# Folding the state into the first-layer weights for two batches at once, with the raw weights streamed through a ring

## What is computed

```python
scores = x @ state.T / 8;   a  = softmax(scores);   xread = a @ state
scores2 = state @ x.T / 8;  a2 = softmax(scores2);  sread = a2 @ x
t = concat([xread, sread], axis=2)       # 544 rows a batch, 4352 in all, width 512
y = ((t @ w_a) * (t @ w_b)) @ w_out      # w_a, w_b: 512 x 1536, w_out: 1536 x 512
e = argmax(y @ w_gate)                   # one of 8 experts for each row
out = softmax(y @ w_gate)[e] * (relu(y @ w1[e]) @ w2[e])
```

## Time and profile before

| what | us |
|---|---|
| median of 3 runs | 1473.31 |
| lowest and highest run | 1472.83, 1474.9 |
| span of the profiled execution, first to last instruction | 1464.0 |
| first stage in the trace, to the start of the state batch | 836.7 |
| share of the span that PE is busy | 95% |
| share of the span for DVE, ACT, POOL | 43%, 38%, 20% |

### The profile page before, as it was taken

One profiled execution on the slowest core, in us unless ns is written; L12 is line 12 of the kernel. 1 busy time (PEld: TensorE's weight loads), 2 busy tenths in 40 slices (PEclk: granted clock), 3 DMA queues, 4 the chain that ended last, 5 costly groups with the idle time before them and its releaser, 6 DMA issues.

```text
span 1464.0 us, 22574 instructions
## 1 busy us (share of the span) xinstructions
PE 1398.0 (95%) x6994; PEld 1160.4 (79%) x6995; DVE 630.3 (43%) x978; ACT 551.8 (38%) x920; POOL 287.3 (20%) x277
## 2 busy tenths in 40 slices
PE   6999999999999999999999996799999999999996
PEld 4688888888888888888888795688787888888885
DVE  4566566566565565666665547211111111111110
ACT  2344545445444544544454532122222222222221
POOL 0000222221221322222222321111111111111120
PEclk9999999999999999999999997699999999999998
DMA  7101543444344334435344556851677774171110
GB/s 240 44 22 65 175 142 133 158 136 153 135 149 162 128 131 170 138 126 180 125 158 144 189 187 205 260 167 43 206 251 257 248 255 157 60 255 43 43 38 0
DMA packets 127087, 215.17 MB, mean 147 GB/s; under 512 B 47760, under 2 KB 47760, under 8 KB 127056
## 3 DMA queue, kind: packets, MB, share of 16 engines
q1 hardware_dynamic: 115888, 186.70, 38.4%
q0 software_dynamic: 6560, 19.67, 4.0%
q10 hardware_dynamic: 4608, 8.39, 1.6%
HBM read 129.78 MB, written 86.77 MB: 148 GB/s over the span
## 4 chain that ended last, share of the span: by engine, by line
PE 72%; DMA 16%; DVE 5%; ACT 2%; issue 2%; SPq 1%; POOL 1%; DVEq 0%; ACTq 0%; POOLq 0%
PE YB L1172 15%; PE OB L1298 12%; PE HB L1285 12%; DMA WS<-expert_halves 11%; PE BB L1158 7%; PE AB L1158 7%; PE FB L1133 7%; DMA expert_halves<-raw 3%; DMA raw<-in_moe_w 2%; PE FB L1113 2%; PE FB L1094 2%; PE HT L1307 2%; PE FB L1142 2%; POOL raw L509 1%; PE FB L1138 1%
## 5 line engine op out<-in xcount | busy, mean ns | idle before, releaser
L509 POOL TENSOR_TENSOR raw<-raw,hi 128x512 f32<-128x512 f32 x128 | 190.6, 1499 | 702.1 <-ACT hi L688 702.1
L1285 PE MATMUL HB<-WS,xgh 128*128 x656 | 210.5, 402 | 6.7 <-DMA WS<-expert_halves 6.7
L1298 PE MATMUL OB<-WS,hth 128*128 x656 | 206.6, 396 | 4.0 <-DVE htl L1058 2.8
L1058 DVE TENSOR_TENSOR htl<-HT,hth 128x1024 fp32r<-128x1024 f32 x41 | 50.2, 1225 | 299.4 <-ACT hth L715 299.4
L1172 PE MATMUL YB<-WOh,gh 128*128 128x512 f32 x408 | 163.1, 400 | 1.3 <-ACT y_sb L634 0.6
L1172 PE MATMUL YB<-WOh,gl 128*128 128x512 f32 x408 | 159.9, 392 | 0.0
L1172 PE MATMUL YB<-WOl,gh 128*128 128x512 f32 x408 | 159.2, 390 | 0.0
L1158 PE MATMUL BB<-ATh,SWB 128*128 128x512 f32 (+1 forms) x432 | 152.2, 388 | 0.0
L1158 PE MATMUL AB<-ATh,SWA 128*128 128x512 f32 (+1 forms) x432 | 150.0, 383 | 2.0 <-ACT gp L657 2.0
L1285 PEld LDWEIGHTS HB<-WS,xgh 128*128 128x128 f32 x656 | 122.9, 192 | 32.5 <-issue 7.7
L1298 PEld LDWEIGHTS OB<-WS,hth 128*128 128x128 f32 x656 | 120.3, 188 | 28.8 <-issue 5.1
(11 more groups left out here) (187 smaller groups left out, 2389.1 us busy)
## 6 DMA issues: line engine op xcount, KB each, us to landing
WS<-expert_halves SPq DMA_DIRECT2D x128, 512.0 KB
raw<-in_moe_w SPq DMA_DIRECT2D x128, 256.0 KB, 2.7
expert_halves<-hi SPq DMA_DIRECT2D x128, 256.0 KB, 2.5
expert_halves<-raw SPq DMA_DIRECT2D x128, 256.0 KB, 2.9
y_rows<-y_sb ACTq DMA_DIRECT2D x32, 256.0 KB, 2.9
xq<-in_x SPq DMA_DIRECT2D x60, 128.0 KB, 2.9
WA<-in_moe_w_a SPq DMA_DIRECT2D x3, 1024.0 KB, 9.9
WB<-in_moe_w_b SPq DMA_DIRECT2D x3, 1024.0 KB, 12.0
```

The source lines that it names most:

```text
L509: eng.tensor_tensor(raw[:, q % 2, :], raw[:, q % 2, :], hi[:, q % 2, :].bitcast(F32), ALU.subtract).then_inc(s["e_lo"], 1)
L1058: eng.tensor_tensor(htl[:, :, :], HT[:, :, :].rearrange("p a (k c) -> p (a k) c", c=P), hth[:, :, :].bitcast(F32), ALU.subtract).then_inc( ...
L1285: last = eng.matmul(HB[:, i, :], act[:, k, :], w, start=(k == 0 and m == 0), stop=(k == KC - 1 and m == 2))
L1298: last = eng.matmul(OB[:, :], act[:, k, :], w, start=(k == 0 and m == 0), stop=(k == FEC - 1 and m == 2))
```

## The change

It does five things. (1) The state of two batches (a *pair*) is laid into one block: chunk k now gives 2 batches x 2 heads x 32 = 128 useful rows. A fold is one chunk, 3 matmuls, and its result is copied to both batches' part of `SW` in two ops of 64 partitions on ACT and two on DVE; a pair takes 24 folds. (2) `WA`, `WB` are gone; each fold's 128x512 chunk of raw weights is loaded when needed into the two-slot ring `wr` (12 slots `wfirst` in the preamble). SP issues each of these loads in order among its others, after waiting until the chunk that held the slot has been split. (3) Pair 0 is folded in float32: 8 folds in the preamble, 16 in batch 0. (4) The preamble no longer runs a2t and sr of batch 0; they move into its steps 0 and 1. (5) xt copies move from DVE to ACT, the softmax of scores is cut in three (shift, exp, normalise) and spread, the product with BB is taken one place earlier on DVE. The raw weights for the state batch also come through the ring. The loop over batches is written out.

```diff
-    state_v = state.rearrange("b (g i) n d -> b i n g d", i=4)
-    wa_v = w_a.rearrange("(k p) (j c) -> j p k c", p=P, c=512)
-    wb_v = w_b.rearrange("(k p) (j c) -> j p k c", p=P, c=512)
+    state_v = state.rearrange("(q r) (g c i) n d -> r c i n q g d", r=2, c=2, i=2)
+    w_v = [w.rearrange("(k p) (j c) -> j k p c", p=P, c=512) for w in (w_a, w_b)]
...
-        lows = ExitStack()
-        WL = [sb(n, [P, KC, FF], F32R, lows) for n in ("WAL", "WBL")]
-        lows.close()
-        W = [sb(n, [P, KC, FF], F32, first) for n in ("WA", "WB")]
-        SW = [sb(n, [P, FC, 2 * G, P], F32R, first) for n in ("SWA", "SWB")]
...
+        SW = sb("SW", [P, FJ, 2, 2, 4, 2 * G, P], F32R, first)
...
-        wfh, wfl = (sb(n, [P, 2, 512], F32R, heads) for n in ("wfh", "wfl"))
+        wfh, wfl = (sb(n, [P, 512], F32R, heads) for n in ("wfh", "wfl"))
+        wr = sb("wr", [P, 2, 512], F32, heads)
...
-        REST = {(0, 3): ("fold", 8), (1, 3): ("fold", 9), (2, 3): ("fold", 10), (3, 3): ("fold", 11)}
-        HEADS = {(4, 0): ("st", 0), (4, 1): ("xt", 0), (4, 2): ("xt", 1), (4, 3): ("fold", 0), (5, 0): ("st", 1),
-                 (5, 2): ("s1", 0), (5, 3): ("fold", 1), (6, 2): ("s2", 0), (6, 3): ("fold", 2),
-                 (7, 1): ("a2t", 0), (7, 2): ("sr", 0), (7, 3): ("fold", 3), (8, 2): ("xt", 2), (8, 4): ("xt", 3),
-                 (8, 3): ("fold", 4), (9, 1): ("s1", 1), (9, 2): ("s2", 1), (9, 3): ("fold", 5),
-                 (10, 1): ("a2t", 1), (10, 2): ("sr", 1), (10, 3): ("fold", 6),
-                 (11, 1): ("a1t", 0), (11, 2): ("a1t", 1), (11, 3): ("fold", 7)}
+        HEADS = {(4, 0): ("xt", 0), (4, 2): ("xt", 1), (5, 0): ("s1", 0), (5, 2): ("s2", 0), (6, 2): ("a2t", 0),
+                 (7, 0): ("sr", 0), (8, 0): ("xt", 2), (8, 2): ("xt", 3), (9, 0): ("s1", 1), (9, 2): ("s2", 1),
+                 (10, 2): ("a2t", 1), (11, 0): ("sr", 1), (11, 1): ("a1t", 0), (11, 2): ("a1t", 1)}
+        BEGIN = {(0, 0): ("a2t", 0), (0, 2): ("sr", 0), (1, 0): ("a2t", 1), (1, 2): ("sr", 1)}
+        NORM = {(6, 4): 0, (10, 4): 1}
+        FOLD_BEGIN = ((0, 1), (0, 3), (1, 1), (1, 3), (2, 1), (2, 3), (3, 0), (3, 1),
+                      (3, 3), (4, 1), (4, 3), (5, 1), (5, 3), (6, 1), (6, 3), (7, 1))
+        FOLD_ODD = ((4, 1), (4, 3), (5, 3), (6, 1), (6, 3), (7, 1), (7, 3), (8, 3), (9, 1), (9, 3), (10, 1), (10, 3))
+        FOLD_EVEN = ((0, 3), (1, 1), (1, 3), (2, 1), (2, 3), (3, 1), (3, 3), (4, 3), (5, 1), (5, 3), (6, 3), (7, 1))
...
+        PER_PAIR = FJ * 2 * KC
+        FOLDS = PAIRS * PER_PAIR
+        PRE = (("st", 0, 0), ("xt", 0, 0), ("xt", 1, 0), ("xt", 2, 0), ("xt", 3, 0), ("s1", 0, 0), ("s1", 1, 0),
+               ("s2", 0, 0), ("s2", 1, 0), ("a1t", 0, 0), ("a1t", 1, 0))
+
+        RING = 16
...
+        def folds_of(b):
+
+            if b == 0:
+                return {k: KC * 2 + i for i, k in enumerate(FOLD_BEGIN)}
+            if b % 2:
+                return {k: PER_PAIR * (b // 2 + 1) + i for i, k in enumerate(FOLD_ODD)}
+            return {k: PER_PAIR * (b // 2) + 12 + i for i, k in enumerate(FOLD_EVEN)}
...
+        def splits_of(b):
+            return {k: v - FOLDS for k, v in folds_of(b).items()} if b >= B - 1 else {}
...
+        def ring_free(i):
+
+            a = RING + i
+            if a < PER_PAIR:
+                return s["fill_done"], next(n for n, e in enumerate(ORDER) if e[:2] == ("fold", a)) + 1
+            if a < FOLDS:
+                return s["wf_lo"], a - PER_PAIR + 1
+            return s["ws_lo"], a - FOLDS + 1
...
+            def load_ring(slot):
+
+                for i in range(2, RINGS):
+                    if used_at(i - 2) == slot:
+                        eng.wait_ge(*ring_free(i - 2))
+                        load_raw(RING + i)
...
-            bodies(eng, emit)
...
-                        for q in pieces_of(b, f):
-                            load_piece(b, q)
-                            if q and not (isinstance(b, int) and b == 0 and q == LEAD):
-                                store_piece(b, q - 1)
-                if expert_in(b):
-                    store_piece(b, pieces_of(b, FC - 1)[-1])
-
-            bodies(eng, emit)
+                    for place in range(2):
+                        if (f, place) in slots:
+                            load_ring(slots[f, place] - RING)
+                    for q in pieces_of(b, f):
+                        load_piece(b, q)
+                        if q and not (b == 0 and q == LEAD):
+                            store_piece(b, q - 1)
+                    for place in range(2, PLACES):
+                        if (f, place) in slots:
+                            load_ring(slots[f, place] - RING)
+                store_piece(b, pieces_of(b, FC - 1)[-1])
             store_y(eng, B, 0)
...
+            def high_folded(a, bank):
+                p, j, m, k = fold_of(a)
+                for side in range(2):
+                    r = rows_of(side, k)
+                    eng.activation(SW[r, j, side, m, :, 2 * (k // 2), :], bank[r, :].rearrange("p (f c) -> p f c", c=P),
                                    ACT.Copy).then_inc(s["sw_hi"], 1)
-                    if not (isinstance(b, int) and b < 0 and a < 7) and not last_fold(a, b):
-                        high_fold(*next_fold(a, b)[:2], b)
-
-            def high_fold(j, w, b):
-                if isinstance(b, int) and b < 0:
-                    eng.wait_ge(w_in[j], 32)
-                eng.activation(wfh[:, :, :], w, ACT.Copy).then_inc(s["wf_hi"], 1)
+
+            def high_fold(a):
+
+                src, done, value = raw_piece(a)
+                eng.wait_ge(done, value)
+                eng.activation(wfh[:, :], src, ACT.Copy).then_inc(s["wf_hi"], 1)
+
+            def fold(a, n):
+                eng.wait_ge(s["fill_done"], n + 1)
+                high_folded(a, FB[:, n % 2, :])
+                if PER_PAIR <= a + 1 < FOLDS:
+                    high_fold(a + 1)
...
+            def split(i):
+                _, j, m, k = fold_of(i)
+                src, done, value = raw_piece(FOLDS + i)
+                eng.wait_ge(done, value)
+                eng.wait_ge(s["b_done"], (B - 2 + m) * FC + 4 * j + 4)
+                eng.activation(state_part(j, m, k, 0), src, ACT.Copy).then_inc(s["ws_hi"], 1)
 
...
+            def low_folded(a, bank):
+                p, j, m, k = fold_of(a)
+                for side in range(2):
+                    r, c = rows_of(side, k), 2 * (k // 2)
+                    place = SW[r, j, side, m, :, :, :]
+                    eng.wait_ge(s["sw_hi"], 2 * a + side + 1)
+                    eng.tensor_tensor(place[:, :, c + 1, :], bank[r, :].rearrange("p (f c) -> p f c", c=P),
+                                      place[:, :, c, :].bitcast(F32), ALU.subtract).then_inc(s["sw_lo"], 1)
+
+            def low_fold(a):
+                src, _, _ = raw_piece(a)
+                eng.wait_ge(s["wf_hi"], a - PER_PAIR + 1)
+                eng.tensor_tensor(wfl[:, :], src, wfh[:, :].bitcast(F32), ALU.subtract).then_inc(s["wf_lo"], 1)
+
+            def fold(a, n):
+                low_folded(a, FB[:, n % 2, :])
+                if PER_PAIR <= a + 1 < FOLDS:
+                    low_fold(a + 1)
+
+            def split(i):
+                _, j, m, k = fold_of(i)
+                src, _, _ = raw_piece(FOLDS + i)
+                eng.wait_ge(s["ws_hi"], i + 1)
+                eng.tensor_tensor(state_part(j, m, k, 1), src, state_part(j, m, k, 0).bitcast(F32), ALU.subtract)\
...
+            def fold(a, bank):
+
+                p, j, m, k = fold_of(a)
+                if p == 0:
+                    src, done, value = raw_piece(a)
+                    eng.wait_ge(done, value)
+                    return eng.matmul(bank, st[:, k, :], src, start=True, stop=True)
+                eng.wait_ge(s["stl_ready"], p + 1)
+                eng.wait_ge(s["wf_lo"], a - PER_PAIR + 1)
+                for i, (part, w) in enumerate(((sth, wfh), (sth, wfl), (stl, wfh))):
+                    last = eng.matmul(bank, part[:, k, :], w[:, :], start=(i == 0), stop=(i == 2))
+                return last
```

751 lines of the change are left out of this document (387 added, 364 removed).

## The result

| | us | against before |
|---|---|---|
| before, median | 1473.62 (1472.83 to 1474.9) | |
| changed, median | 1498.62 (1492.48 to 1503.66) | ratio 1.017, 95% interval 1.0142 to 1.0199 |
| changed, profiled execution | 1492.48, span 1490.7 | |

A forecast was written before the change was run, and what follows sets the result against it. PE was taken to bound batches 1 to 6. Against the 1464.0 us span, -7.8 (preamble, batch 0), -51.6 (matmuls), +17.4 (stalls), -4.3 (batch 7) and +1.5 (state batch) gave 1419; 9.3 carried over made 1428.5, range 1408 to 1454.

The forecast's parts named there:

- theory A: In the follow-ups: SP's load order makes ACT wait for `raw`, delaying folds; reordering was to save 15 to 30 us.
- what the stalls of batches 1 to 6 cost: Batches 1 to 6: new PE waits from SP's order, DVE in step 10 and fold misses, taken as 17.4 us.
- from W + 7.5: Even batches, step 2: the second piece lands 7.5 us after the `wf_lo` wait ends at W; PE waits 2.9 us.
- Step 5: Even batches, a two-piece step behind a ring load, with one fold in the next step: PE waits 1.7 us.
- I put 0.5 us a batch for the misses: Batches 1 to 6: `wfl` is ready at 6.1, PE wants it at 6.2; it just fits, 0.5 us a batch.
- Both stay under 75% of 92 us: Batches 1 to 6: ACT and DVE, after trading copies, stay busy for under 75% of each batch's 92 us.
- Rival 2: Stalls twice as large, from the DVE and POOL lock or a halved PE clock: 1448 us typical, 1454 worst; chance 0.25.
- Nothing else.: Whole kernel: 24 MB more are read with DMA engines 43% busy, no cost added; the second stage starts the same way.
- Batch 7 and what follows: Batch 7 takes 75.5 us (-4.3), between 72 and 80; splits in the state batch's own steps add 1.5, 0 to 5.
- Rival 3: Slower: in batches 1 to 6 each of 72 folds makes PE wait 1.2 us for `wfl`; 1497 us, chance 0.06.
- the SP term: Even batches, steps 2 and 5: ring loads ahead of pieces cost 4.6 us a batch, 13.8 in three.
- The lock between DVE and POOL: Two-input DVE ops and POOL ops reading SBUF exclude each other; it could add up to 0.9 us to `wfl`.

The follow-up runs named there:

- the kernel with full copies: The reordered kernel with one full-height copy on ACT and one full-height subtraction on DVE per fold instead of two halves each: 1439.66 us, ratio 0.9814 to before.
- the reordered kernel: The changed kernel with SP issuing the piece loads ahead of the ring loads in every step: 1454.07 us, ratio 0.9905 to before.
- the run with only the six places: The changed kernel with piece loads ahead of ring loads only in steps 2 and 5 of batches 2, 4 and 6: 1474.75 us, ratio 1.0031 to before.
- folds in float32: The changed kernel with all folds in plain float32, without the copy to `wfh` and subtraction to `wfl`: 1448.84 us, ratio 0.9862 to before.

## Why the prediction was wrong

**What held.** The preamble: forecast 43.5, measured 41.3, within the few us by which two traces of one preamble differ. PE's own work: 92.6 a batch, measured 92.7. The signs for theory A were there as forecast: waits of PE for `wfl` in step 3 of even batches (3.7, 3.9 and 5.8 us for "some 3"), ACT idle for the load of `raw` just before. And half-height DVE ops take 0.69.

**The step that failed: what the stalls of batches 1 to 6 cost, 17.4 us in the forecast.** They cost 57.2 us of waiting and, with the clock at 0.98, another 11.5 (567.8 us busy for the 556.3 us that the kernel with full copies, at 1.00, was busy). That is 51.3 of the 52.6 us by which the stretch was missed. The odd batches took 102.2 us on average where "about 94" was forecast, the even ones 106.3 for "about 97.5". (The forecast's own parts, 13.8 + 2.4 + 3.0, make 19.2; it took 17.4 without a reason.) The term was mis-sized in these places:

1. *The chain "from W + 7.5"*. The forecast let the store take 2.33 us to the next load, "up to 3". It took 3.43, 3.73 and 5.43 in batches 2, 4 and 6, and 3.57, 3.56 and 3.32 at the same place of the reordered kernel. The 2.33 was read where the stores go alone; at these places of the changed kernel a ring load and a piece load go with them (see the last section). Step 5, forecast at 1.7, shows in step 7, as waits of 1.1 to 1.4 us for `gp` and 1.1 to 1.2 for `xt` that the reordered kernel doesn't have. The place was right, the price was not: 13.8 forecast, 18.2 in the even batches by the run with only the six places, 24.5 by the full reordering.
2. *"I put 0.5 us a batch for the misses"* in the fold chain. This is the larger error. The forecast counted B's end, the fold, two copies, `wfh`, two low parts and `wfl` against 6.2 us, found 0.1 us of room and called it a fit. It left out what else stands in the queues between these ops, and priced the normalisation in step 10 alone, though the change puts one at (6, 4) too. Step 7 of batch 1 shows it, in the timelines of DVE and PE of the changed kernel between the folds at (7, 1) and (7, 3). ACT begins the two copies of the fold's result at 201.62, so the first half lies ready for DVE at about 202.2:

```profile
201.77 0.69 DVE L810 TENSOR_TENSOR s1g<-s1g,small 128x512 f32<-128x512 f32 x1
202.49 0.46 DVE L854 COPY sread<-FB 64x64 f32<-64x64 f32 x2
202.98 0.69 DVE L902 TENSOR_TENSOR gp<-gp,BB 128x512 f32<-128x512 f32 x1
203.70 1.41 DVE L769 TENSOR_TENSOR SW<-FB,SW 64x512 fp32r<-64x512 f32 x2
205.03 0.67 DVE L775 TENSOR_TENSOR wfl<-wr,wfh 128x512 fp32r<-128x512 f32 x1
205.85 0.47 PE L1201 MATMUL FB<-wfh,sth 128*128 128x512 f32 x1 [1.52 <-DVE wfl L775]
```

   A normalisation, the copies of `sread` and the product with BB come first on DVE, and PE waits 1.52 us. The odd batches show this without any help from SP's order: 4.9 to 5.2 us of waits for `wfl`, 1.7 to 2.3 for `sread` behind it. Full-height copies take 25.8 us out of the reordered kernel, where the forecast had 2.4 for step 10 and 3.0 for the misses.
3. *"Both stay under 75% of 92 us"*. True (ACT was busy 320 of 625 us, DVE 344), and no protection: the price of an op on these engines is in its place in a chain. The half copies in the kernel before show it most plainly: 25 us by medians, 29 by span, 15 of them in a stretch where DVE had 39% and ACT 52% of the time to spare.
4. *The clock.* Rival 2 named it; the sum held nothing for it. Windows of 0.97, 0.97 and 0.95 in batches 2, 4 and 6 are its sign. It fell not only behind the long waits in step 3: in batch 2 it was at the lower level, 0.50, from 322.0 to 325.2 us too, right after the 3.1 us of waiting for x, and in batch 0 from 113.7 to 117.0 after 2.2 us.

**"Nothing else."** The load of x was given no cost. PE waits 9.3 us for it in the six batches. It is part of the 57.2. **Batch 0** was forecast at 98.3 and took 103.1. The forecast's parts (16.6 off, 14.2 and 4.4 on) make 2.0 and not the 1.5 that it wrote; beside that stand 2.9 us of waits, for which it had no term, and a granted clock of 0.96 (1.00 before), about 4 us by that figure. Together they are more than the 4.8 us of the miss.

**Batch 7 and what follows.** Forecast -4.3 and +1.5, measured +1.9 and +11.7. Of the 11.7, 7.4 lie in the state batch's first layer (61.9 us from its first matmul to its last into `AB`, 54.5 before) and 4.3 behind it. The forecast named the mechanism for batch 7 ("the splits through the ring put SP's waits before loads") and then let PE's own work decide. The reordering gives batch 7 back 6.8 us and lands at 74.9, which is the forecast's 75.5; it gives the rest 10.1 us, 6.0 of them in the state batch's first layer.

**The rivals.** Rival 3 was priced at 1497 and the result was 1498.6, but its mechanism, a wait at each of 72 folds, is not what the trace shows; there are 18. What happened is rival 2's (stalls twice as large and the clock) at twice rival 2's size (51.3 us above the sum against its 25), in batches 1 to 6, and the SP term in batch 7 and the state batch. The lock between DVE and POOL, which rival 2 also named, did not hit `wfl`: all 72 of them ran 671 to 695 ns. It hit POOL instead. In 26 cases `wfl` and POOL's subtraction overlapped; each time `wfl` had started first, by 0.1 to 0.4 us, and POOL's op took 1.44 to 1.75 us, where nearly all others of batches 1 to 6 took 1.26 to 1.31. One such pair, the changed kernel:

```profile
301.99 0.67 DVE L775 TENSOR_TENSOR wfl<-wr,wfh 128x512 fp32r<-128x512 f32 x1
302.06 1.75 POOL L497 TENSOR_TENSOR raw<-raw,hi 128x512 f32<-128x512 f32 x1 [8.93 <-ACT hi L640]
```

By the Trainium skill, page "SBUF — State Buffer", section "SBUF: two separate sides", whichever of a DVE op with two SBUF inputs and a POOL op that reads SBUF starts first holds the other off; the trace agrees.

**What stays open.** Order and chain overlap by 22 us of 83, so the miss can't be split between them in one way. Of the extra 11.7 us behind the state batch's start, the part in its first layer hangs on SP's order. Batch 7 and that layer together took 143.5 to 143.7 us in the three kernels that keep the changed order there (changed, only where priced, folds in float32), 130.7 to 132.7 in the five with the pieces first, and 134.3 before (137.6 with the loop written out). Which of the loads costs it was not tried. The 4.3 us behind it are not shown to be the change's: that stretch, whose second stage no kernel changes, took 572.2 to 578.7 us over the kernels whose rows go to the same experts. The 9.3 us that the forecast carried over from span to median is not a property of the kernel: in every later profiled execution the device time is 1.7 to 2.0 us above the span, so that of before took some 1466 us, and a forecast against the median has to say by how much the profiled execution was faster than usual.

## What to carry to other kernels

In a queue that runs in order, put a load whose issue waits for a compute result behind the loads that don't; here the wait was otherwise paid by the engine that stood at the later load, and moving the waiting loads to another engine's queue gave less than reordering. When a chain fits its slot by 0.1 us, price the miss of each round by what else its engines run between its links, not by their share of busy time. And before an op is split by partitions, count ops: on DVE and ACT an op of 64 partitions took as long as one of 128.
